# Bucketed attention, routed experts and an ELU block on one core: q and k handed over head dimension first, fp32 projection in four 32-column products

## The chip, the cores and the metric

The kernel runs on one core of one Trainium2 chip. The metric is the device time of one execution in microseconds (us). Lower is better. Profiles come from one execution of their own, which has a time and, inside it, a span from the first to the last profiled instruction.

## What is computed

Three stages follow one another. The change touches the first.

```
# attention: batch 2, 8 heads, 768 tokens, head dimension 64; proj is 64 x 6
q_bits = (einsum('bhsd,dk->bhsk', q, proj) > 0);  k_bits likewise
q_bucket = sum(q_bits * 2**arange(6));            k_bucket likewise
mask   = q_bucket[:, :, :, None] == k_bucket[:, :, None, :]
scores = where(mask, q @ k.T / 8, -1e9)
attn   = exp(scores - max) / (sum + 1e-9)
out    = attn @ v
# then: 1536 tokens routed to one of 8 experts (512 -> 1024 -> 512, relu, two gates)
# then: x @ w_in (2048 wide), ELU, @ w_out
```

A query sees only the keys of its own bucket, so each sign of a projection matters: it is worked out to fp32 precision.

## The kernel before

**Attention, head by head.** There are 16 heads (batch times heads). A head's 768 tokens are six tiles of 128. Six scores tiles `m` are made per head, each 128 queries by 768 keys in two halves of 384 columns, into the PSUM pairs `pair_s` and `pair_t` in turn (`scores`, four products of 384 columns). DVE takes the row maximum (`row_max`), ACT the exponential (`exp_rows`), PE turns the result in six 128x128 transposes into `pair_u` (`turn_exps`), ACT and DVE copy half of it each (`copy_t0`, `copy_t1`), and `times_v` multiplies with v. `times_v` is fp32 and its stationary operand has 64 columns: two heads' halves go to columns 0 to 63 and 64 to 127 of the array, product by product in turn, and each fp32 product shows as two records in the profile. `last` turns the result back and multiplies the routing gates in.

**Masks.** The bucket mask rides in the scores product: rows 64 to 127 of `q_a` and `k_a` hold a one-hot code of the bucket (of `k_a` times 2^60), rows 0 to 63 hold q and k. The second pair, `q_b` and `k_b`, adds what rounding to the fast fp32r format took away: high part times low part.

**Preparation of a head before the change.** q and k arrive token first. PE turns them (`turn_qk`, three transposes each of q and k) into the 384 columns of a bank, with even tiles in partitions 0 to 63 and odd ones in 64 to 127. ACT makes the high part (`split_hi`), DVE the low part (`split_lo`), POOL copies both to where the scores need them (`place_hi`, `place_lo`, ten copies of 64x384). PE projects (`project`: two fp32r products of 128 columns each for q and for k), ACT moves half of it (`keep_low`), DVE compares with zero (`sign`), PE makes the code (`code`), DVE and ACT write the mask rows (`mask_even`, `mask_odd`).

**Order.** Every engine has its queue written out by hand, in groups `n`, three per head (`part` 0, 1, 2). In group `n` stand the scores of `m_s = 2(n-3)` and `m_s+1`, the turning of `m_e = 2(n-4)` and `m_e+1`, the preparation of head `g = n//3` and the `times_v` of the head two back. An instruction waits for semaphores; what stands behind it on its engine waits with it. Heads 0 and 1 are prepared ahead of the loop. In groups 24 to 47, DVE also makes the high part of the first expert's weights (line 1003), and POOL the low part (`w_lo`). SP issues the loads and the stores of the rows.

**After attention** come routing (one chain of small steps), 19 slots of expert products, and the ELU block. The change leaves all this as it was, but for one wait and for the bank in which the last head's rows stand.

Of the kernel before, what the change touches and what calls it, by code (L numbers as in the profile page):

```python
# [22 lines left out]
ALU = mybir.AluOpType  # L23
# [8 lines left out]
P = 128  # L32
# [36 lines left out]
COPIES = 5  # L69
WARM_UP = (7, 6)  # L70
# [13 lines left out]
_WIDTHS = [("ident", P), ("popcount", 1), ("unmatched", 1), ("minus_pop", 1), ("pattern", P), ("tri", P), ("ones", P),  # L84
# [11 lines left out]
def constants():  # L96
# [11 lines left out]
    pattern = np.zeros((P, P))  # L108
    for side in range(2):
        pattern[side * BIT_K:side * BIT_K + NBITS, side * BUCKETS:(side + 1) * BUCKETS] = 2.0 * bits - 1.0  # L110
    put("pattern", pattern)
# [16 lines left out]
def program(nc, q, k, v, proj, w_gate, w_ogate, w1, w2, w_in, w_out, const, out):  # L128
    with ExitStack() as ctx:
# [31 lines left out]
        with ExitStack() as att:  # L161
# [10 lines left out]
            raw = sb("raw", [P, 2, 2, J, D])  # L172
            q_a = sb("q_a", [P, 2, S], F32R)
            k_a = sb("k_a", [P, 2, S], F32R)
            q_b = sb("q_b", [P, 2, S], F32R)
            k_b = sb("k_b", [P, 2, S], F32R)
            x_lo = sb("x_lo", [P, 2, HALF], F32R)
            bits = sb("bits", [P, 2, HALF], BF16)
            nmax = sb("nmax", [P, 2, J])
            proj2 = sb("proj2", [P, NBITS])  # L180
            pat = sb("pat", [P, P])
            pat_bf = sb("pat_bf", [P, P], BF16)
            proj_w = sb("proj_w", [P, 3, P], F32R)
            low_sb = sb("low_sb", [P, 2, HALF])
# [75 lines left out]
        u_bank = lambda u: bank_a if u == HEADS else bank_b  # L260
# [19 lines left out]
        prep_bank = lambda u: bank_b if u in (1, 3) else bank_a  # L280

        def tiles(x, g, odd):
            return x[:, g % 2, :].rearrange("p (j two n) -> p two j n", two=2, n=P)[:, odd]

        def turned(bank):
            return bank[:, 0:HALF].rearrange("p (j n) -> p j n", n=P)
# [3 lines left out]
        s_raw = [[sem(f"s_raw{i}{x}") for x in "qk"] for i in range(2)]  # L290
        s_vld = [sem(f"s_vld{i}") for i in range(4)]
        s_setup = sem("s_setup")
        s_tqk = sem("s_tqk")
        s_hi = sem("s_hi")
        s_lo = sem("s_lo")
        s_cp, s_cpa = sem("s_cp"), sem("s_cpa")
# [4 lines left out]
        s_low = sem("s_low")  # L301
        s_code = sem("s_code")
        s_both = sem("s_both")
        s_pwh, s_pw = sem("s_pwh"), sem("s_pw")
# [89 lines left out]
        copies = lambda u: COPIES * max(u, 1) + 1  # L394
# [4 lines left out]
        def _(sp):  # L399
# [8 lines left out]

            def load_head(g):
                if g >= 5:  # L410
                    store_rows(g - 5)
                if g >= 2:
                    sp.wait_ge(s_tqk, 2 * (g - 2) + 2)
                for n, x in enumerate((q, k)):
                    sp.dma_start(raw[:, g % 2, n], rows(x, g)).then_inc(s_raw[g % 2][n], 16)
                if g >= 4:
                    sp.wait_ge(s_av, g - 2)
                if g >= 2:
                    load_v(g)

            def load_v(g):
                sp.dma_start(v_nat[:, g % 4], rows(v, g)).then_inc(s_vld[g % 4], 16)

            load_head(0)
            sp.dma_start(pat[:, :], const[:, slice(*COL["pattern"])]).then_inc(s_pat, 16)
            load_head(1)
            sp.dma_start(cst[:, P:], const[:, P:]).then_inc(s_cst, 16)
            load_v(0)
            load_v(1)
# [17 lines left out]
            for u in range(HEADS - 5, UNITS):  # L447
                store_rows(u)
# [20 lines left out]
        def _(pool):  # L469
# [24 lines left out]
            def place_hi(g, c):  # L494

                u = 2 * g + c
                if g >= 2:
                    pool.wait_ge(s_sc, J * (g - 1))
                if g >= 3:
                    pool.wait_ge(s_x, g - 2)  # L500
                pool.wait_ge(s_cp, copies(u - 1))
                pool.wait_ge(s_hi, u + 1)
                if c == 0:
                    hi = tiles(q_b, g, 0).bitcast(F32)
                    pool.tensor_copy(tiles(q_b, g, 1)[0:D], hi[D:P]).then_inc(s_cp, 1)
                    pool.wait_ge(s_cp, copies(u - 1) + 1)
                    pool.tensor_copy(tiles(q_a, g, 1)[0:D], hi[D:P]).then_inc(s_cp, 1)
                    pool.wait_ge(s_cp, copies(u - 1) + 2)
                    pool.tensor_copy(tiles(q_a, g, 0)[0:D], hi[0:D]).then_inc(s_cp, 1)
                else:  # L510
                    hi = tiles(k_b, g, 1).bitcast(F32)
                    pool.tensor_copy(tiles(k_b, g, 0)[D:P], hi[0:D]).then_inc(s_cp, 1)
                    pool.wait_ge(s_cp, copies(u - 1) + 1)
                    pool.tensor_copy(tiles(k_a, g, 0)[0:D], hi[0:D]).then_inc(s_cp, 1)
                    pool.wait_ge(s_cp, copies(u - 1) + 2)
                    pool.tensor_copy(tiles(k_a, g, 1)[0:D], hi[D:P]).then_inc(s_cp, 1)

            def place_lo(g, c):

                u = 2 * g + c  # L520
                lo = turned(x_lo[:, c, :]).bitcast(F32)
                pool.wait_ge(s_lo, u + 1)
                pool.wait_ge(s_cp, copies(u) - 2)
                if c == 0:
# [1083 lines left out]
```

## Time and profile before

| | |
|---|---|
| time, median of 3 runs | 789.18 us (788.76 to 789.18) |
| profiled execution: time, and its span | 789.62 us, 787.8 us |
| attention (to the first routing step) | about the first 261 us of the span |
| PE busy over the span | 98% |
| DVE, ACT, POOL busy over the span | 58%, 47%, 43% |

The time is the span and about 1.8 us around it. PE's busy share is high all along the span; whether another engine makes it wait is seen only in the chain of waits and in the small gaps, not in the share.

### The profile page before, as it was taken

How to read it: one execution, taken by the hardware profiler on the slowest of the kernel's cores; microseconds unless marked ns; L12 is line 12 of the kernel's file. 1: busy time of each engine (PE TensorE's matmuls, PEld its weight loads, DVE VectorE, ACT ScalarE, POOL GpSimd, SP SyncE). 2: the span in 40 equal slices, each digit the busy share in tenths (PEclk: the TensorE clock that was granted, in tenths of full speed). 3: DMA queues.
4: the chain of work that ended last, by engine and by line, in shares of the span. 5: the costliest groups of instructions: out<-in, count | busy, mean ns of one | idle time of the engine just before them, and what ended most of it. 6: DMA issues, size and time to landing. Idle time of an engine off the chain costs nothing.

```text
span 787.8 us, 12747 instructions
## 1 busy us (share of the span) xinstructions
PE 772.6 (98%) x4269; PEld 646.3 (82%) x4269; DVE 453.6 (58%) x805; ACT 372.9 (47%) x702; POOL 340.7 (43%) x340
## 2 busy tenths in 40 slices
PE   8999999999999899999999999999999999999997
PEld 6777777787776688888888888899899889989985
DVE  7877878888885655454454544669336316513720
ACT  6787887888776243224432340057227206503610
POOL 4344344656562389798777981134210010000000
PEclk9999999999999999999999999999999999999999
DMA  6022332321110288567465640530010010000000
GB/s 200 22 64 68 110 92 68 88 62 41 42 32 21 50 300 271 182 230 239 154 222 172 229 161 28 174 121 1 28 53 1 14 54 14 0 14 28 1 14 27
DMA packets 41805, 72.68 MB, mean 92 GB/s; under 512 B 18768, under 2 KB 25168, under 8 KB 41744
## 3 DMA queue, kind: packets, MB, share of 16 engines
q10 hardware_dynamic: 9456, 31.53, 12.2%
q1 hardware_dynamic: 28848, 29.06, 11.8%
q0 software_dynamic: 3440, 11.28, 4.3%
q8 instruction: 38, 0.62, 0.3%
q14 instruction: 23, 0.19, 0.1%
HBM read 60.57 MB, written 11.28 MB: 91 GB/s over the span
## 4 chain that ended last, share of the span: by engine, by line
PE 63%; issue 28%; DVE 4%; POOL 2%; ACT 2%; DMA 0%; POOLq 0%; DVEq 0%; ACTq 0%
PE pair_s L1480 13%; PE pair_t L1495 13%; PE bank_b L1305 8%; PE pair_u L1290 7%; PE pair_s L1279 5%; PE pair_t L1279 4%; PE pair_u L1459 2%; PE bank_a L1243 2%; PE bank_b L1325 1%; PE bank_a L1257 1%; POOL out L642 1%; PE pair_s L1532 1%; DVE g_lo L1222 1%; PE bank_a L1265 1%; POOL y_raw L636 1%
## 5 line engine op out<-in xcount | busy, mean ns | idle before, releaser
L472 POOL TENSOR_TENSOR w_part<-w_raw,w_part 128x1024 fp32r<-128x1024 f32 x80 | 190.1, 2414 | 57.4 <-ACT w_part L750 56.7
L750 ACT ACTIVATE w_part<-w_raw 128x1024 fp32r<-128x1024 f32 x72 | 73.8, 1054 | 133.8 <-PE pair_t L1495 101.2
L1582 PE MATMUL pair_t<-w_part,g_hi 128*128 128x512 f32 x384 | 118.9, 391 | 0.3 <-POOL w_part L472 0.3
L1480 PE MATMUL pair_s<-w_part,xs_t 128*128 x456 | 108.7, 394 | 0.3 <-DVE xs_t L1100 0.3
L1495 PE MATMUL pair_t<-w_part,hid_t 128*128 x456 | 109.0, 394 | 0.0
L642 POOL DMA_INDIRECT out<-o_sb,token x12 | 11.8, 986 | 208.5 <-DVE o_sb L1192 208.5
L1480 PEld LDWEIGHTS pair_s<-w_part,xs_t 128*128 128x128 f32 x456 | 84.3, 188 | 17.6 <-issue 0.8
L1495 PEld LDWEIGHTS pair_t<-w_part,hid_t 128*128 128x128 f32 x456 | 84.4, 189 | 16.8
L857 ACT ACTIVATE elu<-elu 128x384 f32<-128x384 f32 x64 | 33.6, 525 | 123.1 <-DVE elu L1212 122.9
L1582 PEld LDWEIGHTS pair_t<-w_part,g_hi 128*128 128x128 f32 x384 | 71.6, 188 | 15.1 <-issue 0.7
L1290 PE MATMUL pair_u<-first,exps 128*128 128x128 f32 x564 | 77.5, 273 | 0.3 <-ACT exps_t L708 0.2
L1582 PE MATMUL pair_t<-w_part,g_lo 128*128 128x512 f32 x192 | 74.9, 390 | 0.0
L1532 PE MATMUL pair_u<-y_t,w_part 128*128 128x384 f32 x384 | 69.3, 334 | 0.3 <-DVE elu L1217 0.3
L1532 PE MATMUL pair_s<-y_t,w_part 128*128 128x384 f32 x384 | 69.3, 335 | 0.0
L1290 PEld LDWEIGHTS pair_u<-first,exps 128*128 128x128 f32 x564 | 65.9, 141 | 3.2 <-ACT exps L699 1.0
L1532 PEld LDWEIGHTS pair_u<-y_t,w_part 128*128 128x128 f32 x384 | 66.8, 188 | 0.7 <-DVE elu L1217 0.6
L1532 PEld LDWEIGHTS pair_s<-y_t,w_part 128*128 128x128 f32 x384 | 66.9, 188 | 0.2
L1305 PE MATMUL bank_b<-exps_t,v_nat 128*64 128x384 f32 x360 | 64.7, 494 | 0.9 <-ACT rows_sb L731 0.9
L1118 DVE CAST hid_t<-pair_u 128x512 fp32r<-128x512 f32 x38 | 26.0, 685 | 67.2 <-PE pair_u L1459 67.2
L903 DVE TENSOR_REDUCE nmax<-pair_s 128x1 f32<-128x768 f32 x48 | 45.8, 954 | 18.0 <-PE pair_s L1279 17.0
L932 DVE COPY exps_t<-pair_u 128x384 f32<-128x384 f32 x94 | 51.5, 548 | 6.4 <-PE pair_u L1290 5.8
L708 ACT ACTIVATE exps_t<-pair_u 128x384 f32<-128x384 f32 x94 | 46.0, 489 | 13.0 <-PE pair_u L1290 11.3
(233 smaller groups left out, 1208.8 us busy)
## 6 DMA issues: line engine op xcount, KB each, us to landing
w_raw<-in_moe_w ACTq DMA_DIRECT2D x48, 512.0 KB, 6.1
w_raw<-in_moe_w SPq DMA_DIRECT2D x16, 512.0 KB, 5.5
ys_sorted<-ys SPq DMA_DIRECT2D x19, 256.5 KB, 3.4
w_raw<-in_moe_w_in ACTq DMA_DIRECT2D x8, 512.0 KB, 6.6
raw<-in_q SPq DMA_DIRECT2D x16, 192.0 KB, 3.8
raw<-in_k SPq DMA_DIRECT2D x16, 192.0 KB, 3.7
v_nat<-in_v SPq DMA_DIRECT2D x16, 192.0 KB, 2.6
x_rows<-rows_sb SPq DMA_DIRECT2D x32, 96.0 KB, 2.4
```

Source lines behind the costliest of these rows:

```text
L472: pool.tensor_tensor(chunk_of(w_part, n, 1, c), w_raw[n % 2][c][:, :], chunk_of(w_part, n, 0, c).bitcast(F32), ALU.subtract).then_inc(s_wl ...
L708: act.activation(turned_tile(m, slice(0, JH)), exps_pair(m)[:, 0, 0:HALF].rearrange("p (j n) -> p j n", j=JH), ACT.Copy).then_inc(s_t0, 1)
L750: act.activation(chunk_of(w_part, n, 0, c), w_raw[n % 2][c][:, :], ACT.Copy).then_inc(s_whi, 1)
L903: dve.tensor_reduce(nmax[:, g % 2, qt:qt + 1], score_pair[m % 2][:, :, 0:HALF], AX.XY, ALU.max, negate=True).then_inc(s_mx, 1)
L932: dve.tensor_copy(turned_tile(m, slice(JH, J)), exps_pair(m)[:, 1, 0:HALF].rearrange("p (j n) -> p j n", j=JH)).then_inc(s_t1, 1)
L1279: mm = pe.matmul(score_pair[m % 2][:, h, 0:HALF], a[:, g % 2, t], b[:, g % 2, h * HALF:(h + 1) * HALF], start=first, stop=not first)
L1290: mm = pe.transpose(exps_pair(m)[:, part, n * P:(n + 1) * P], exps[:, m % 4, kt * P:(kt + 1) * P], ident)
L1305: mm = pe.matmul(u_bank(u)[o * D:(o + 1) * D, 0:HALF], v_nat[:, (u - 1 + o) % 4, j, :], turned_half(2 * u - 1 + o)[:, j], start=j == 0, st ...
L1480: mm = pe.matmul(pair_s[:, h, :], xs_t[:, xp, c * P:(c + 1) * P], w_part[:, bass.ds(par, 1), wp, a:a + 512], start=c == 0 and xp == 0 and ...
L1495: mm = pe.matmul(pair_t[:, s % 2, :], hid_t[:, hp, c * P:(c + 1) * P], w_part[:, bass.ds(par, 1), wp, a:a + DM], start=c == 0 and n == 0, ...
L1532: mm = pe.matmul(hidden_bank[n % 4][:, 0:NB], w_in_p[:, wp, c, f * P:(f + 1) * P], y_t[:, yp, c, :], start=c == 0 and m == 0, stop=c == CD ...
L1582: mm = pe.matmul(pair_t[:, t % 2, :], gp[:, f, j * P:(j + 1) * P], w_out_p[:, wp, f, :], start=f == 0 and m == 0, stop=f == FT - 1 and m == 2)
```

## The change

q and k are handed to the kernel transposed, head dimension in front and tokens in the order that the tiles want (`x.reshape(B, H, P, J, D).transpose(0, 1, 4, 3, 2)`). SP loads each of them twice per head, to partitions 0 to 63 and to 64 to 127. The transposes on PE, and `split_hi`, `split_lo` and `keep_low`, are gone. DVE makes the high parts of q and k in one copy of 128x768 each (`high`); POOL scales k (`raw`, 128x768), copies two high parts and subtracts two low parts (64x768 each). The projection is four plain fp32 products with a 32-column stationary operand and 64 rows, one each for the halves of q and k, into partitions 0, 32, 64 and 96 of one bank; one `sign` follows for q and k together. `q_a`, `k_a`, `q_b` and `k_b` have three buffers in place of two. `scores` of a group stand together in all three parts. The high part of the first expert's weights goes from DVE to ACT in halves. The last head's unit has `bank_a`.

```
-            raw = sb("raw", [P, 2, 2, J, D])
-            q_a = sb("q_a", [P, 2, S], F32R)
-            x_lo = sb("x_lo", [P, 2, HALF], F32R)
+            raw = sb("raw", [P, 2, 2, S])
+            q_a = sb("q_a", [P, 3, S], F32R)
...
-            def turn_qk(g, c):
-                for n in range(JH):
-                    mm = pe.transpose(prep_bank(u)[:, n * P:(n + 1) * P], raw[:, g % 2, c, 2 * n:2 * n + 2, :].rearrange("p j d -> p (j d)"),
-                                      ident)
...
-                parts = ((0, hi), (1, hi), (0, lo)) if g <= 1 else ((2, hi), (0, lo))
-                for n, (w, x) in enumerate(parts):
-                    mm = pe.matmul(prep_bank(u)[:, 0:HALF], proj_w[:, w, :], x, start=n == 0, stop=n == len(parts) - 1)
+            def project(g):
+                    masks = {1: 2, 2: 3}
+                    pe.wait_ge(s_ks, g)
+                    pe.wait_ge(s_raw[g % 2][0], 16 * (g // 2 + 1))
+                    pe.wait_ge(s_mq, masks[g] if g in masks else 2 * g)
+                    pe.wait_ge(s_mk, masks[g] if g in masks else 2 * g)
+                for i in range(4):
+                    mm = pe.matmul(bank_a[i * BIT_K:(i + 1) * BIT_K, 0:HALF], proj_w[:, :],
+                                   raw[0:D, g % 2, i // 2, i % 2 * HALF:(i % 2 + 1) * HALF], start=True, stop=True)
+                mm.then_inc(s_bits, 1)
...
+            def load_qk(g, n, to):
+                sp.dma_start(raw[to, g % 2, n], (q, k)[n][g // H, g % H]).then_inc(
+                    (s_raw if to == top else s_low)[g % 2][n], 16)
...
+            def place_q(g):
+                pool.wait_ge(s_ks, g)
+                pool.wait_ge(s_hia if g == 1 else s_hi, 2 if g == 1 else 2 * (g - 2) + 1)
+                pool.tensor_copy(q_a[top, g % 3, :], q_b[top, g % 3, :].bitcast(F32)).then_inc(s_cp, 1)
+                pool.wait_ge(s_cp, prepared(g - 1) + 1)
+                pool.tensor_tensor(q_b[low, g % 3, :], raw[low, g % 2, 0, :], q_b[low, g % 3, :].bitcast(F32),
+                                   ALU.subtract).then_inc(s_cp, 1)
...
+                pool.tensor_scalar(raw[:, g % 2, 1, :], raw[:, g % 2, 1, :], SCALE, None, ALU.mult).then_inc(s_ks, 1)
+                place_q(g)
+                place_k(g)
...
+            def high(g, c):
+                dve.tensor_copy((q_b, k_b)[c][:, g % 3, :], raw[:, g % 2, c, :]).then_inc(s_hi if g else s_hid, 1)
...
+            def sign(g):
+                dve.wait_ge(s_bits, g + 1)
+                dve.tensor_scalar(bits[:, :], bank_a[:, 0:HALF], 0.0, None, ALU.is_gt).then_inc(s_sgn, 1)
...
-                    if 1 <= u < HEADS:
+                    if 1 <= u < HEADS - 1:
                         pe.wait_ge(s_fr, u)
...
+            pe.wait_ge(s_x, HEADS)
```

**PE's queue, groups of one head.** The head whose `times_v` stands here is in its first and second part; `L1257` is the projection, `L1243` the turning of q or k, `L1265` the code, `L1305` is `times_v`. From the third part of the head before to `times_v`, before the change:

```order
L1325 MATMUL bank_b<-last_w,u_sb 128x160 x3
L1290 MATMUL pair_u<-first,exps 128x128 x6
L1243 MATMUL bank_a<-first,raw 128x128 x3
L1279 MATMUL pair_s<-k_a,q_a 128x384 x2
L1279 MATMUL pair_s<-k_b,q_b 128x384 x2
L1279 MATMUL pair_t<-k_a,q_a 128x384 x2
L1279 MATMUL pair_t<-k_b,q_b 128x384 x2
L1290 MATMUL pair_u<-first,exps 128x128 x6
L1257 MATMUL bank_a<-q_b,proj_w 128x384
L1257 MATMUL bank_a<-x_lo,proj_w 128x384
L1305 MATMUL bank_b<-exps_t,v_nat 64x384 x6
L1265 MATMUL bank_a<-bits,pat_bf 128x384
```

The same place after the change, where `L1155` is the projection of q and k:

```order
L1228 MATMUL bank_b<-last_w,u_sb 128x160 x3
L1191 MATMUL pair_u<-first,exps 128x128 x6
L1155 MATMUL bank_a<-raw,proj_w 32x384 x4
L1180 MATMUL pair_s<-k_a,q_a 128x384 x2
L1180 MATMUL pair_s<-k_b,q_b 128x384 x2
L1180 MATMUL pair_t<-k_a,q_a 128x384 x2
L1180 MATMUL pair_t<-k_b,q_b 128x384 x2
L1191 MATMUL pair_u<-first,exps 128x128 x6
L1206 MATMUL bank_b<-exps_t,v_nat 64x384 x6
L1191 MATMUL pair_u<-first,exps 128x128 x6
L1166 MATMUL bank_a<-bits,pat_bf 128x384
```

The four projection products stand where the turning stood, between two products of the whole array, and the code has moved behind the second turning of the part.

**DVE's queue, second and third part of a head, after the change** (`L860` is `copy_t1`, `L838` is `row_max`, `L831` is `high` of k for the next head, `L852` is `mask_even`, `L866` and `L867` are `inverse`):

```order
L860 COPY exps_t<-pair_u 128x3x128
L838 TENSOR_REDUCE nmax<-pair_s 128x1
L838 TENSOR_REDUCE nmax<-pair_t 128x1
L860 COPY exps_t<-pair_u 128x3x128
L831 CAST k_b<-raw 128x768
L852 TENSOR_SCALAR k_a<-bank_a,first 64x384
L866 TENSOR_SCALAR den<-den 128x6
L867 RECIPROCAL den<-den 128x6
L860 COPY exps_t<-pair_u 128x3x128
L838 TENSOR_REDUCE nmax<-pair_s 128x1
L838 TENSOR_REDUCE nmax<-pair_t 128x1
L860 COPY exps_t<-pair_u 128x3x128 x2
```

Before the change the low part (`L895`), the sign (`L915`) and the mask stood at these places, and a row maximum of the third part was drawn into the second.

**POOL's queue, one head after the change** (`L532` scales k, the next four lines are `place_q` and `place_k`, the last three `rows_of`):

```order
L532 TENSOR_SCALAR raw<-raw 128x768
L505 CAST q_a<-q_b 64x768
L507 TENSOR_TENSOR q_b<-raw,q_b 64x768
L514 CAST k_a<-k_b 64x768
L516 TENSOR_TENSOR k_b<-raw,k_b 64x768
L488 TENSOR_TENSOR rows_sb<-rows_sb,den 128x6x16
L495 TENSOR_TENSOR logit<-logit,rows_sb 128x96
L496 TENSOR_TENSOR rows_sb<-rows_sb,den 128x6x64
```

Before, ten copies of 64x384 stood in the place of the first five, and `rows_of` stood ahead of them.

## Rows read from the trace of the kernel before

**Rows 1.** The page: span; busy time, its share, instructions.

```profile
span 787.8 us, 12747 instructions
PE 772.6 (98%) x4269; PEld 646.3 (82%) x4269; DVE 453.6 (58%) x805; ACT 372.9 (47%) x702; POOL 340.7 (43%) x340
```

**Rows 2.** Chain that ended last, within attention: start us, length us, engine, line.

```profile
21.88 0.98 PE pair_s L1279 x4
...
36.49 0.52 PE bank_a L1243 x3
...
206.80 0.70 PE pair_s L1279 x4
...
208.19 0.66 PE pair_u L1290 x6
208.85 0.35 PE bank_a L1257 x2
209.20 2.09 PE bank_b L1305 x12
211.29 0.27 PE bank_a L1265
...
213.63 0.33 PE bank_a L1243 x3
...
216.70 0.90 PE pair_s L1279 x4
...
219.29 0.28 PE bank_a L1265
...
220.24 0.82 PE bank_b L1325 x6
...
221.72 0.52 PE bank_a L1243 x3
...
241.52 0.81 PE pair_u L1290 x6
```

**Rows 3.** Busy time by engine, one head's period.

```profile
206.28:221.72 15.44, 15.44 (x104) 11.78 (x103) 12.74 (x21) 12.34 (x27) 9.20 (x14) 1.00 0.11 28
```

**Rows 4.** Timeline of one `times_v`: its first weight loads, its products.

```profile
214.54 0.20 PEld L1305 LDWEIGHTS bank_b<-exps_t,v_nat 128*64 128x64 f32 x4 [0.17 <-issue]
214.54 2.16 PE L1305 MATMUL bank_b<-exps_t,v_nat 128*64 128x384 f32 x12
```

**Rows 5.** Timeline: a DVE copy within SBUF and the POOL copies beside it.

```profile
215.83 0.50 POOL L516 CAST k_a<-k_b 64x384 fp32r<-64x384 f32 x1
215.94 0.94 DVE L1003 CAST w_part<-w_raw 128x1024 fp32r<-128x1024 f32 x1
216.46 0.78 POOL L527 CAST k_b<-x_lo 64x384 fp32r<-64x384 f32 x1
```

**Rows 6.** Groups by line: count, busy us, mean ns, idle before.

```profile
L472 POOL TENSOR_TENSOR w_part<-w_raw,w_part 128x1024 fp32r<-128x1024 f32 x80 | 190.1, 2414 | 57.4 <-ACT w_part L750 56.7
L491 POOL TENSOR_TENSOR rows_sb<-rows_sb,den 128x384 f32<-128x384 f32 x14 | 11.6, 831 | 0.0
L708 ACT ACTIVATE exps_t<-pair_u 128x384 f32<-128x384 f32 x94 | 46.0, 489 | 13.0 <-PE pair_u L1290 11.3
```

**Rows 7.** Timeline: two row maxima, one behind the other.

```profile
208.00 0.95 DVE L903 TENSOR_REDUCE nmax<-pair_s 128x1 f32<-128x768 f32 x1
208.86 0.95 DVE L903 TENSOR_REDUCE nmax<-pair_t 128x1 f32<-128x768 f32 x1
```

**Rows 8.** Timeline of the end of attention.

```profile
251.07 0.56 ACT L731 ACTIVATE rows_sb<-bank_b 128x480 f32<-128x480 f32 x1
251.78 2.16 PE L1305 MATMUL bank_b<-exps_t,v_nat 128*64 128x384 f32 x12 [0.87 <-ACT rows_sb L731]
260.91 1.33 ACT L744 ACTIVATE rows_sb<-bank_b,den 128x64 f32<-128x64 f32 x6 [0.95 <-DVE lg_part L1015]
263.26 0.22 PE L1426 MATMUL bank_a<-onehot,tri_bf 128*128 128x104 bf16 x1
```

More of the change, by code:

```diff
@@ L68 @@
 GROUP_S, GROUP_E = 3, 4
-COPIES = 5
-WARM_UP = (7, 6)
+COPIES = 4
+WARM_UP = (7, 10)
 BIT_K = 32
@@ L107, in constants @@
     bits = (np.arange(BUCKETS)[None, :] >> np.arange(NBITS)[:, None]) & 1
[L108 to L111, printed above, removed]
+    pattern = np.zeros((P, 2, P))
+    for x in range(2):
+        for side in range(2):
+            a = (2 * x + side) * BIT_K
+            pattern[a:a + NBITS, x, side * BUCKETS:(side + 1) * BUCKETS] = 2.0 * bits - 1.0
+    put("pattern", pattern.reshape(P, 2 * P))
     put("popcount", np.tile(bits.sum(0), 2)[:, None])
@@ L391, in load_ends @@
                     for e in range(first, last)}
-        copies = lambda u: COPIES * max(u, 1) + 1
+        prepared = lambda g: COPIES * g + 1
         shares = lambda u: 2 * (u + 1)
@@ L553, in _ @@
[L553 to L573 removed]
+            top, low = slice(0, D), slice(D, P)
@@ L584, in _ @@
                         pool.wait_ge(s_twice, 2 + o)
-                if g >= 9:
-                    pool.wait_ge(s_cp, copies(2 * g + 1))
-                    w_lo(0, g - 9)
-            pool.wait_ge(s_cp, copies(2 * HEADS - 1))
-            for c in range(HEADS - 9, NCH):
-                w_lo(0, c)
-            for g in range(HEADS - 3, HEADS - 1):
-                rows_of(g)
+                if g >= 4:
+                    rows_of(g - 4)
+                if g >= 10:
+                    w_lo(0, g - 10)
+            rows_of(HEADS - 4)
+            w_lo(0, HEADS - 10)
+            rows_of(HEADS - 3)
+            w_lo(0, HEADS - 9)
+            rows_of(HEADS - 2)
             pool.wait_ge(s_reach, 1)
@@ L963, in _ @@
             row_max(3)
-            sign(1, 1)
+            high(2, 1)
+            sign(1)
             copy_t1(1)
@@ L1390, in _ @@
                     turn_exps(m_e)
-                if g < HEADS and part == 0:
-                    project(g, 0)
                 if n == 3 * HEADS + 3:
                     turn_exps(m_e + 1)
-                if g == 2 and part == 0:
+                if g < HEADS and part == 1:
+                    code(g, 1)
+                if g == 2 and part == 1:
                     times_v_alone(0, 0, 0)
@@ L1398, in _ @@
                     times_v(g - 2, part)
-                if part == 1 and m_s + 2 < J * HEADS:
-                    scores(m_s + 2)
                 if n == 3 * HEADS + 4:
```

429 lines of the change are left out of this document (150 added, 279 removed).

## The prediction

> **What bounds the kernel now.** I read the page first: PE is busy for 772.6 us of a span of 787.8 us [rows 1]. That alone does not say that PE is never kept waiting, so I took the chain of waits through attention next. From head to head it repeats: the turning of the next q stands at 36.49 us, and twelve heads later at 221.72 us [rows 2], so a head takes (221.72 - 36.49) / 12 = 15.44 us. In one such head DVE has 12.74 us of work, ACT 12.34 and POOL 9.20, at a granted clock of 1.00 [rows 3]. The chain there is PE's rows end to end: PE bounds attention, and what is taken off PE's queue is gained, as long as DVE and ACT deliver in time.
>
> The parts of a head on PE, from [rows 2]: six scores tiles at 0.70, six turnings of exponentials at 0.66, two `times_v` at 2.09, `last` 0.82; for the preparation two turnings of q and k at 0.52 and 0.33, two projections at 0.35, two codes at 0.27 and 0.28. Some of these hold a wait. Four products of 384 columns take 0.70, so one takes 0.17: each code row has 0.10 too much. The turning of 0.52 has 0.19 more than the one of 0.33. And the scores behind a `times_v` take 0.90, not 0.70: leaving the 64-column shape costs 0.20 before scores, 0.10 before a code, and 0.15 before transposes (0.81 against 0.66, the row at 241.52). Sum: 6x0.70 + 6x0.66 + 2x2.09 + 0.82 + 0.85 + 0.70 + 0.55 + 0.20 = 15.46, against 15.44.
>
> **What is removed.** Per head, the turnings with their wait, 0.85, and the projections, 0.70. The code of k stood 0.28 where 0.17 is its work; its sign is now made a part earlier, so 0.11 of wait goes. Together 1.66 us.
>
> **What is added on PE.** Four fp32 products of 384 columns, each in a column group of its own. This shape isn't in the trace; `times_v` is its nearest row. Its six products are twelve records. The stretch of 2.16 us ends with the last record's own length (the group's mean is near 0.49), so the starts spread over 1.67 us: 1.67 / 5 = 0.33, so five steps, six moments; and the weights of four records are loaded at once, within 0.20 us, so that the second group need not wait for the first [rows 4]. Twelve records at six moments is two at each: the two column groups run side by side from the first record on, 0.32 per half product (0.17 x 2 for a product of twice the passes). One product costs 0.64, alone or beside its neighbour; `times_v` is 3 x 0.64 = 1.92 and 0.17 for entering. By this row the bounds for the four products are 0.64 (all side by side) and 4 x 0.64 = 2.56 (none). I take 0.64, since nothing in the row shows the second group paying for the first. With 0.17 for entering and 0.20 for leaving into scores [rows 2], the projection costs 1.01 us a head; the bounds are 1.01 and 2.93. The Trainium skill (TensorEngine Tiling (Array Packing), Key Properties) says that a change of tiling mode drains the engine, which speaks against one more visit per head; the 0.17 and the 0.20 are what this trace shows of it, and they are in the sum.
>
> Leaving `times_v` costs 2 x 0.15 (transposes follow) in place of 0.10 + 0.20: nothing.
>
> **What could newly keep PE waiting.** I laid DVE's and ACT's queues beside PE's for one head: a row maximum starts 0.86 behind the one before it [rows 7], a copy of 384 columns takes 0.49 on ACT [rows 6], and I take 0.55 on DVE. Two places are tight. First, the masks of q wait for the code, which now closes the first part; behind `mask_odd` in ACT's queue stands the copy that the next part's first turning needs. The mask is an ACT instruction of the copy's size: with some 0.15 for each of three hand-overs, 0.17 + 2 x 0.49 + 0.45 = 1.6 us pass from the code's start, against 0.17 + 1.40 of code and scores on PE. I charge 0.06. Second, the third part has little work on PE: from the end of its first scores, DVE does two row maxima and a copy before the second turning's last half can start, against scores 0.70, turning 0.66, `last` 0.82 and half a turning 0.33 = 2.51 on PE. The DVE side is 0.2 to start, 0.86, 0.86 [rows 7] and 0.55 = 2.47. I charge nothing, but any extra work on DVE there goes into PE's time.
>
> DVE's own sum: two low parts and one of two signs (0.55 each, 384 columns) go, two copies of 128x768 come. A 128x1024 copy took 0.94 [rows 5], so each lies between nothing and 0.94; either end leaves DVE's 12.74 us near or under where it was [rows 3]. ACT loses four copies of 384 columns, 0.49 each [rows 6], and gains two of 512 columns in eight heads. POOL: two subtractions of 64x768, between 0.83 and 2.41 each (the 384 and the 1024 column rows) [rows 6], say 1.8; two copies, between 0.50 [rows 5] and 1.0; the scaling, between 0.50 and 2.41, say 1.0; `rows_of` 1.6 (0.83 of it for the 384 columns [rows 6]) and in eight heads `w_lo` 2.4. That is 10.6 us with the middle values and 13.2 with the upper ones, under the 14.9 of a head. It is work for the head after next's scores, so POOL hides behind PE. SP's extra loads have a whole head of room.
>
> The copy at 215.94 and POOL's copy at 216.46 show one more thing: POOL's took 0.78 where its like took 0.50, and it ended 0.36 after DVE's did; DVE's in turn began while POOL's 0.50 was running [rows 5]. One waits for the other. The Trainium skill (SBUF — State Buffer, section on the engine ports) says that DVE and GpSimd share a port pair by exclusive lock; the trace agrees, by the 0.28. In the new order POOL waits for DVE's `high` of q and again of k before it goes on, so they seldom meet. I charge nothing here; it is a rival.
>
> **The sum.** Per head: 15.44 - 1.66 + 1.01 + 0.06 = 14.85, a gain of 0.59. Heads 2 to 14 stand ahead of a projection in the loop: 13 x 0.59 = 7.7 us. In head 15's period no next head is prepared: before, that saved 0.52, now it saves 1.01, so it gains 1.1. At the end, `times_v` of the last unit waited 0.87 us for `copy_rows` to free its bank [rows 8]; it has a bank of its own now, which gives 0.9. The new wait ahead of the routing product costs nothing: ACT's rows end at 262.24, the product starts at 263.26 [rows 8]. It would cost if those rows came over 1 us later.
>
> At the start, the loop's first scores begin at 21.88 us [rows 2]. Now the projection needs only the loads and its weights and no turning, but behind it DVE and POOL pass four instructions of 64x768 or 128x768 to each other before scores can begin, and twice the bytes are loaded. The bounds are 1.5 us sooner (no turning, no splitting) and 2 us later (two POOL subtractions exposed in head 1). I take 0.3 sooner.
>
> Sum: 7.7 + 1.1 + 0.9 + 0.3 = 10.0 us, so the profiled execution goes from 789.62 to 779.6 us. It was 0.44 above the median of 789.18, so the median comes to 779.2; some waits of 0.05 or so that I could not see are likely, and I say 780.0.
>
> **The rivals.**
> - *Column groups wait for one another in program order (slower).* The two halves of a fp32 product stand ahead of the next group's first half. If halves start only in order, the four products take 5 steps of 0.32 = 1.6 us, not 0.64: 13 x 0.96 = 12.5 more, 792.5 us. It decides against the change from 0.64 + 10.0/13 = 1.4 us a projection on. Against it: by the same rule `times_v` would have seven starting moments and spread 6 x 0.32 = 1.92 us, and it spreads 1.67 [rows 4]. For it: only two groups are seen there, not four. The Trainium skill (TensorE: Matmul & The Clock Gate, Part 3) states this rule, that products start and end strictly in program order; the row speaks against it. Chance 0.11. If none run side by side at all, 2.56 each, it is 25 more: 805 us, chance 0.03. Two at a time, 1.28 each: 8.3 more, 788.3 us, chance 0.04.
> - *The DVE copies meet POOL's instructions.* A copy held until a POOL subtraction ends costs up to 1.8; where it falls in the second part, DVE has 0.4 us to spare before its row maximum is due in the third. Some 0.3 to 0.5 a head would come back: 13 x 0.4 = 5, 785 us. For it: the 0.28 of [rows 5]; against: POOL waits for these very copies. Chance 0.13.
> - *The start is worse than thought.* Head 1's low parts are late and the loop starts 2 us later: 782.5 us. Chance 0.09.
> - My forecast, 777 to 783: chance 0.60.
>
> **How the numbers follow.** A measurement of this kernel tells about 0.2%, 1.6 us, from no change. Faster, under 787.6: forecast, port and start, 0.82, less a little for port and start together: 0.81. The two-at-a-time case falls within 0.2%: 0.05. Slower: 0.14. The range from 776 to 788 holds the forecast, the port and the start, and leaves the slower case out (0.14) and a little below.
>
> **What would show it.** In the trace after: a head's period of 14.85 us between two projections; eight records of the projection whose starts fall into two moments 0.32 apart; a projection row of about 0.8 in the chain and 0.9 for the scores behind it; no DVE or ACT entries in the chain of a middle head; the `high` copies near 0.5, and POOL's rows under 11 us a head. It is wrong if the projection's starts are spread over five moments or more, if the chain has row maxima in each third part, or if the loop's first scores come after 23 us.

## The result, and the profile after

The changed kernel takes 792.05 us (median, 791.81 to 792.46); the kernel before, run beside it, 789.18. The ratio is 1.0038, 95% interval 1.0025 to 1.005: slower by a small but measurable amount, where 780.0 and faster had been forecast, with 788 as the upper end of the range. The profiled execution took 792.07 us, with a span of 790.3 us, 2.5 more than before [rows 1].

The page after: span, then busy time, its share and instructions.

```profile
span 790.3 us, 12377 instructions
PE 766.2 (97%) x4237; PEld 628.2 (79%) x4237; DVE 440.8 (56%) x776; ACT 352.7 (45%) x658; POOL 374.3 (47%) x258
```

PE has 6.4 us less work than before, as was meant, and the span is longer. So PE waits now where it did not. Where, is seen by cutting attention at places that both chains have.

**The projection is what was forecast.** Windows on PE's records that write `bank_a`, around one projection: stretch, length, busy time and number of records that lie in it, granted clock, DMA share, GB/s.

```profile
178.37:178.42 0.05, 0.04 (x4) 1.00 0.00 0
178.42:178.72 0.30, 0.30 (x4) 1.00 0.00 0
178.72:178.77 0.05, 0.05 (x8) 1.00 0.00 0
```

Four records begin within 0.05 us, none in the next 0.30, and the other four within 0.05 behind that. These are the two moments of the prediction: all four column groups run side by side. In the chain of the changed kernel the head's period is then read from one projection to the next:

```profile
56.71 0.78 PE bank_a L1155 x8
57.49 0.91 PE pair_s L1180 x4
...
64.93 0.16 PE bank_a L1166
...
71.61 0.78 PE bank_a L1155 x8
```

The projection takes 0.78, the scores behind it 0.91, the code 0.16, and the period is 71.61 - 56.71 = 14.90 us against a forecast of 14.85 and 15.44 before [rows 3]. Nothing but PE stands in the chain between them. But only four periods are like this.

**Heads 8 to 14 are not.** Windows of one head's period, early and late, with the columns of [rows 3] (PE, its weight loads, DVE, ACT, POOL, granted clock, DMA share, GB/s):

```profile
56.71:71.61 14.90, 14.90 (x104) 10.70 (x108) 11.55 (x19) 10.34 (x23) 8.70 (x9) 1.00 0.38 109
199.91:215.44 15.53, 15.00 (x103) 10.61 (x102) 11.56 (x19) 11.39 (x24) 11.25 (x9) 1.00 0.07 18
```

The late one is 15.53 us long, 0.09 more than before, and PE is busy for 15.00 of it: 0.53 is waiting. ACT has 1.05 more work, POOL 2.55 more. Neither is near the period. The chain shows which piece of work it is:

```profile
199.91 0.17 PE bank_a L1166
...
200.13 0.58 issue
200.71 0.63 ACT w_part L696
...
201.36 0.50 ACT exps_t L652
...
201.99 0.85 PE pair_u L1191 x6
```

PE makes the code (L1166). ACT waits for it, writes the mask (L630; the chain books its 0.58 us as issue), then converts half a chunk of the first expert's weights (L696, 0.63), then copies the turned exponentials (L652), for which PE's next turning (L1191) waits. The 0.63 stands in the middle of the one place that the prediction had called tight on ACT, and it is there in the eight heads in which weights are converted.

**Head 3.** The chain at the end of the first part of head 3, in a period of 15.91 us (one projection at 40.80, the next at 56.71):

```profile
47.56 1.12 DVE tri_bf L913
...
48.95 0.48 DVE exps_t L860
...
49.48 0.55 PE pair_u L1191 x3
```

Three constants for routing are converted on DVE in this head alone, ahead of the copy that PE's turning waits for. They stood there before too, and head 3 then took as long as any other (its scores and those of head 4 at 37.01 and 52.45 us, 15.44). What has changed is the length of the first of them. Timeline after, then before:

```profile
46.76 1.84 POOL L507 TENSOR_TENSOR q_b<-raw,q_b 64x768 fp32r<-64x768 f32 x1
...
47.56 1.12 DVE L913 CAST tri_bf<-cst 128x128 bf16<-128x128 f32 x1
```

```profile
42.52 0.52 DVE L996 CAST tri_bf<-cst 128x128 bf16<-128x128 f32 x1
```

It begins while POOL's subtraction runs and ends 0.08 us behind it (48.68 against 48.60), as the one before ended 0.08 behind a POOL copy of 0.50 (from 42.46). The other two constants take 0.21 each. So of the 1.0 us that head 3 takes more than the next (15.91 - 14.90), 0.60 is DVE held longer by POOL. The other 0.4 would be the place alone; that split is an estimate.

**The start.** The chain from the loads to the first projection inside the loop's even beat:

```profile
2.61 5.27 DMA pat<-in_const
...
7.93 1.06 POOL pat_bf L520
...
11.78 2.16 POOL raw L532
...
17.88 1.83 POOL k_b L516
...
20.15 2.14 POOL raw L532
...
22.32 0.04 DVE k_b L831
...
22.79 0.55 DVE bits L845
...
27.89 0.80 PE pair_s L1180 x4
...
40.80 0.78 PE bank_a L1155 x8
41.58 0.55 PE pair_s L1180 x2
```

From 7.93 to 22.32 the chain is POOL's rows nearly all the way, with one ACT copy of 0.85 and short hand-overs between them. The scaling of k, put at 1.0 us in the prediction, takes 2.1; DVE's high part of k (L831) waits for the second scaling, and the sign, a copy and a row maximum wait behind it on DVE. The loop's first scores begin at 27.89, not at 21.88 [rows 2]. The forecast had called 23 the point from which it is wrong.

**The end.** `times_v` of the last unit, which had waited 0.87 us [rows 8], follows the turning at once:

```profile
253.55 0.76 PE pair_u L1191 x6
254.31 2.09 PE bank_a L1206 x12
```

**The sum of the differences**, from the two chains at the same instructions (after minus before):

| stretch | forecast | measured |
|---|---|---|
| to the loop's first scores (27.89 against 21.88) | -0.3 | +6.0 |
| head 2, from there to the scores at 41.58 against 37.01 | -0.6 | -1.4 |
| head 3 (15.91 against 15.44) | -0.6 | +0.5 |
| heads 4 to 7 (4 x (14.90 - 15.44)) | -2.4 | -2.2 |
| heads 8 to 14 (7 x (15.53 - 15.44)) | -4.1 | +0.6 |
| head 15 | -1.1 | -0.2 |
| the last units | -0.9 | -0.8 |
| sum | -10.0 | +2.5 |

+2.5 is the difference of the spans. The misses add up to 12.5 us: 5.5 up to head 3, 1.1 in head 3, 0.2 in heads 4 to 7, 4.7 in heads 8 to 14, 0.9 in head 15, 0.1 at the end. Head 15 has a weights conversion too (0.63 at 231.76 in the chain); the other 0.3 there was not traced.

### The profile page after: what moved, and what is told of

Same layout as the page of the kernel before. It is cut to its first block, busy times and chain, and to the rows that moved or that the text cites. A ratio compares the mean times of both kernels' runs of the same rounds, so it can differ in the third digit from the quotient of the medians.

```text
span 790.3 us, 12377 instructions
## 1 busy us (share of the span) xinstructions
PE 766.2 (97%) x4237; PEld 628.2 (79%) x4237; DVE 440.8 (56%) x776; ACT 352.7 (45%) x658; POOL 374.3 (47%) x258
## 4 chain that ended last, share of the span: by engine, by line
PE 59%; issue 28%; DVE 4%; POOL 4%; ACT 2%; DMA 1%; POOLq 0%; SPq 0%; DVEq 0%
PE pair_s L1369 13%; PE pair_t L1384 13%; PE pair_u L1191 8%; PE bank_b L1206 7%; PE pair_s L1180 4%; PE pair_t L1180 3%; PE pair_u L1348 2%; PE bank_b L1228 1%; PE bank_a L1155 1%; POOL out L605 1%; PE pair_s L1421 1%; DVE g_lo L1132 1%; POOL y_raw L599 1%; DMA pat<-in_const 1%; ACT w_part L696 1%
## 5 line engine op out<-in xcount | busy, mean ns | idle before, releaser
L1191 PEld LDWEIGHTS pair_u<-first,exps 128*128 128x128 f32 x564 | 62.7, 140 | 32.4 <-ACT exps L643 18.6
L1191 PE MATMUL pair_u<-first,exps 128*128 128x128 f32 x564 | 81.0, 278 | 6.0 <-ACT exps_t L652 4.6
L652 ACT ACTIVATE exps_t<-pair_u 128x384 f32<-128x384 f32 x94 | 46.0, 489 | 49.9 <-PE pair_u L1191 49.6
L860 DVE COPY exps_t<-pair_u 128x384 f32<-128x384 f32 x94 | 51.8, 552 | 23.8 <-PE pair_u L1191 23.4
L1206 PE MATMUL bank_b<-exps_t,v_nat 128*64 128x384 f32 x336 | 60.4, 494 | 0.0
L838 DVE TENSOR_REDUCE nmax<-pair_s 128x1 f32<-128x768 f32 x48 | 45.8, 954 | 18.9 <-PE pair_s L1180 17.5
```

The costliest lines, as they stand in the source:

```text
L652: act.activation(turned_tile(m, slice(0, JH)), exps_pair(m)[:, 0, 0:HALF].rearrange("p (j n) -> p j n", j=JH), ACT.Copy).then_inc(s_t0, 1)
L838: dve.tensor_reduce(nmax[:, g % 2, qt:qt + 1], score_pair[m % 2][:, :, 0:HALF], AX.XY, ALU.max, negate=True).then_inc(s_mx, 1)
L860: dve.tensor_copy(turned_tile(m, slice(JH, J)), exps_pair(m)[:, 1, 0:HALF].rearrange("p (j n) -> p j n", j=JH)).then_inc(s_t1, 1)
L1191: mm = pe.transpose(exps_pair(m)[:, part, n * P:(n + 1) * P], exps[:, m % 4, kt * P:(kt + 1) * P], ident)
L1206: mm = pe.matmul(u_bank(u)[o * D:(o + 1) * D, 0:HALF], v_nat[:, (u - 1 + o) % 4, j, :], turned_half(2 * u - 1 + o)[:, j], start=j == 0, st ...
```

## The experiments

Three causes were read from the trace. Each of the first three kernels takes one away and nothing else; the fourth takes all three. The kernel before took 788.93 us beside them (788.88 beside experiments 5 to 8, 788.98 beside 9 to 11).

**1. The weights ahead of the mask on ACT** (theory: the place of the 0.63 us costs it; rival: ACT's larger sum of work).

```
+                if 8 <= g < 8 + NCH and part == 0:
+                    first_hi(g - 8, part)
                 if g < HEADS and part < 2:
                     mask_odd(g, part)
                 if g >= 2 and part == 1:
                     copy_u(g - 2)
-                if 8 <= g < 8 + NCH and part < 2:
+                if 8 <= g < 8 + NCH and part == 1:
                     first_hi(g - 8, part)
```

> Changed kernel with one line moved: in heads 8 to 15, ACT makes the first half of a weight chunk's high part ahead of the mask of q (where it sits idle 1.07 us in the first part of a head), not behind it. Theory: that half chunk, 0.63 us, stands in front of the copy that PE's next turning waits for, once a head; so a head's period falls from 15.53 to 14.90 us and the time from 792.05 by 8 x 0.63 = 5.0 to 787.0 us. Rival: ACT simply has too much to do in these heads (11.39 us of 15.53), the place doesn't matter: period 15.4 to 15.5, time 791.5 to 792.

Measured: 787.58 us, ratio to before 0.9982 (0.9973 to 0.9991). 4.5 us came back by moving one ACT instruction in eight heads. Windows of one period of this kernel, with the same columns:

```profile
191.07:206.06 14.99, 14.99 (x105) 10.63 (x108) 11.55 (x19) 11.38 (x25) 11.26 (x10) 1.00 0.33 80
```

ACT and POOL are as busy as in the late row above (11.38 and 11.26), and PE waits for nothing. The place was the cost, not the amount. Head 15, from its first scores to the first behind it, takes 14.21 us (221.84 to 236.05), where the changed kernel took 14.74 (225.83 to 240.57).

**2. DVE's high part of k later in the start** (theory: it drags what stands behind it on DVE through POOL's 2.13 us).

```
             row_max(3)
-            high(2, 1)
             sign(1)
...
             copy_t1(2)
+            high(2, 1)
```

> Changed kernel with one line moved: ahead of the loop DVE makes the high part of head 2's k behind everything else, not ahead of head 1's sign. Theory: that copy waits for POOL's scaling until 22.3 us and holds sign, copy and row maximum behind it (DVE idle 2.30 us, PE 2.10 us); head 1's sign moves from 22.8 to about 20.0 us, the loop's first scores from 27.7 to about 25.0, the time falls by 2.6 to 789.4 us. Rival: POOL's chain (its low parts of head 1 end at 19.7) or the loads set the loop's start, the wait only moves: under 0.8 us gained.

Measured: 789.77 us, ratio 1.0005 (0.9995 to 1.0014), 2.3 us less than the changed kernel. In its chain the first regular projection comes 2.24 us sooner than at 40.80:

```profile
38.56 0.78 PE bank_a L1155 x8
```

**3. The routing constants ahead of the mask on DVE**, where the mask's wait for the code covers them.

```
+                if n == 9:
+                    dve.wait_ge(s_cst, 16)
+                    dve.tensor_copy(tri_bf[:, :], cc("tri"))
+                    dve.tensor_copy(ones_bf[:, :], cc("ones"))
+                    dve.tensor_copy(iota_bf[:, :], cc("iota"))
                 if g < HEADS and part < 2:
                     mask_even(g, part)
-                if n == 9:
...
```

> Changed kernel with three DVE copies of routing constants in head 3 moved ahead of the mask of q, where DVE is idle 1.2 us. Theory: behind the mask they held the copy that PE waits for (0.80 us idle at 49.5): head 3's period falls from 15.91 to 14.9 us, the time by 1.0 to 791.0 us. Rival: the first of them meets POOL's copy wherever it stands (1.12 us where its like before took 0.52), and holds the mask now: period 15.5 to 15.9, time 791.6 to 792.

Measured: 791.44 us, ratio 1.004 (1.0026 to 1.0054). By the times alone that is hardly told from the changed kernel. The trace tells it: head 3's projections stand at 40.75 and 55.66, a period of 14.91 us and not 15.91, so the 1.0 us is gone. The three conversions together still take 1.11 us (45.62 to 46.73), as the last of them now takes 0.84 beside a POOL copy; the mask behind them starts at 46.89, when the code is there, so they hold nothing. From its chain:

```profile
55.66 0.44 PE bank_a L1155
```

**4. All three.**

> Changed kernel with the three moves of the other runs together. Theory: they are in different stretches and add up, 5.0 + 2.6 + 1.0 = 8.6 us: 783.4 us, faster than the kernel before by 0.7%. Rival: one of them only makes room for the next wait; then 785 to 788 us.

Measured: 784.34 us, ratio 0.9945 (0.9932 to 0.9957): 7.7 us less than the changed kernel, where the three alone gave 4.5, 2.3 and 0.6. They add up to 7.4, within the scatter of the runs, so they are separate causes. This kernel is faster than before by 4.6 us. Its scores of the first regular head begin at 39.21: the start is still 2.2 us behind before. The next four went after that.

**5. ACT's table load out of the way**, in the kernel of experiment 4.

```
+            act.wait_ge(s_zero, 3)
+            act.activation(u_sb[0:D, 0:1], last_w[0:D, 0, 1, 0:1], ACT.Copy)
             act.wait_ge(s_raw[0][1], 16)
```

> The kernel of e4_three (784.34 us, first scores at 11.79 us of its trace) with one more ACT instruction of one element ahead of its wait for k, so that the 1.28 us of table load pass while nothing else can be done. Theory (the table load holds the copy k_b, 8.07, but pat_bf on POOL, 7.70 to 8.10, is due at the same time): the first code stays near 8.2, first scores near 11.7, 784.3 us. Rival (the table load alone is what is late): k_b near 6.8, code near 7.0, first scores near 10.5, 783.1 us.

Measured: 784.14 us, ratio 0.9932 (0.9918 to 0.9945); code at 8.43, first scores at 11.97. The load of 1.28 us now passes at 2.87, and k's high part is there 1.3 us sooner, but nothing later moves: the patterns were due at the same time. As the theory had it.

**6. The patterns sooner, and on DVE.** As 5, and:

```
             sp.dma_start(proj_w[:, 0:NBITS], proj).then_inc(s_proj, 16)
-            load_qk(0, 0, low)
             sp.dma_start(pat[:, :, :], const[:, slice(*COL["pattern"])]...
+            load_qk(0, 0, low)
...
-            pool.tensor_copy(pat_bf[:, :, :], pat[:, :, :]).then_inc(s_setup, 1)
...
             sign(0)
+            dve.wait_ge(s_pat, 16)
+            dve.tensor_copy(pat_bf[:, :, :], pat[:, :, :]).then_inc(s_setup, 1)
```

> As s1_table, and the sign patterns are loaded one transfer earlier and cast on DVE, not on POOL. Theory: the table load and the patterns together are what holds the first code; it comes near 7.1, the mask q_a on POOL near 8.8 to 10.4, first scores near 10.7, and the loop starts 1.1 us sooner: 783.2 us. Rival (from the first scores to the loop it is POOL's own scaling of 2.13 us and its subtractions of 1.8 us, which begin with the loads of the low parts and not with the first scores): first scores near 10.7 but the loop's first as in e4_three, 784.3 us.

Measured: 784.06 us, ratio 0.9938 (0.9924 to 0.9951). Neither line of the expectation came out. The code came at 8.18, not 7.1: the cast now stands behind the sign on DVE. Timeline of this kernel:

```profile
7.33 0.71 DVE L872 CAST pat_bf<-pat 128x256 bf16<-128x256 f32 x1
...
8.18 0.48 PE L1169 MATMUL bank_a<-bits,pat_bf 128*128 128x384 bf16 x1 [1.40 <-DVE pat_bf L872]
...
10.91 2.15 POOL L529 TENSOR_SCALAR raw<-raw 128x768 f32<-128x768 f32 x1 [0.73 <-DMA raw<-in_k]
...
11.68 0.62 PE L1183 MATMUL pair_s<-k_a,q_a 128*128 128x384 f32 x2
```

And yet the first regular head's scores began at 38.49, 0.72 sooner than in experiment 4, where the first scores had moved by only 0.11 (11.79 to 11.68). What had moved by 0.72 is POOL's first scaling (11.63 to 10.91). So the loop's start follows POOL's row of work and not the first scores, as far as this one step of 0.72 us shows. The gain does not show in the median. The profiled execution is the slowest of its five (785.62 us); from 250 to 300 us it has a granted clock of 0.97, where experiment 4 has 1.00.

**7 and 8. Two warm-up products in place of ten** ahead of the first scores, in the kernel of experiment 4 and in that of 6 (`WARM_UP = (7, 2)`; the output does not depend on them). The changed kernel has ten of these products there, the kernel before six; this too is part of the change.

> The kernel of e4_three with 2 of the 10 warm-up products ahead of the first scores, not 10 (the output is not touched by them). Theory: they end 0.1 us before the mask of q that the first scores wait for anyway, so nothing is gained by leaving them out, and PE's products after them are spaced wider for longer (0.32 us for one of 384 columns instead of 0.17): 784.3 to 785.3 us. Rival (the warm-up holds the first scores): 783.3 us or less.

Measured: 786.86 us, ratio 0.9968 (0.9956 to 0.9979), 2.5 us above experiment 4: the direction of the theory, and more than its range. Two of the eleven executions (783.41 and 784.29 us) lost nothing. In the profiled one (786.93) the loss is in the start: the first regular projection comes at 41.03 us against 38.43 in experiment 4.

> s2_pat and s3_warm together. Theory: 2.9 us of warm-up would end near 10.6, about when the mask of q is ready, so leaving 8 of them out adds nothing to s2_pat: 783.2 us. Rival (they hold the scores once the patterns come sooner): 0.5 us or more below s2_pat, 782.6 us.

Measured: 785.43 us (783.92 to 787.08), ratio 0.9963 (0.9949 to 0.9976), 1.4 above experiment 6: neither 783.2 nor 782.6. The profiled execution is the fastest of the five and lost nothing (first regular projection at 37.78, 37.72 in experiment 6). Timeline of the second scores, experiment 4 first, then 7:

```profile
15.82 0.58 PE L1182 MATMUL pair_s<-k_a,q_a 128*128 128x384 f32 x2 [2.36 <-ACT exps L643]
...
16.59 0.82 PE L1193 MATMUL pair_u<-first,exps 128*128 128x128 f32 x6
```

```profile
15.80 0.98 PE L1182 MATMUL pair_s<-k_a,q_a 128*128 128x384 f32 x2 [1.12 <-ACT exps L643]
...
17.21 1.49 PE L1193 MATMUL pair_u<-first,exps 128*128 128x128 f32 x6
```

From the start of these four scores products to the start of the turning behind them 0.77 us pass in experiment 4 (16.59 - 15.82) and 1.41 in experiment 7 (17.21 - 15.80), with nothing between them in either. In experiment 7 this lasts until about 20 us; in the profiled execution of experiment 8 it is over with the second scores (0.79 us from 15.53 to 16.32). So the loss differs from execution to execution, and by the medians the warm-up is worth its place, though the first scores start no later with it (11.79 us against 11.77).

**9. The projection's products made twice**, in the changed kernel; the output is the same.

```
-                for i in range(4):
+                for i in (0, 1, 2, 3, 0, 1, 2, 3):
```

> The changed kernel with the four products of every projection made a second time (groups 0, 1, 2, 3 and again 0, 1, 2, 3, the same values into the same places). Theory (column groups run side by side, each group is busy 0.64 us for one fp32 product of 384 columns): the projection's 0.78 us become 1.42, of which little is hidden in heads 4 to 14 (16 projections in all, 15 of them on the path): 10 us more than the changed kernel, 802 us, and all eight projections of the trace's first eight records again start within 0.4 us. Rival (products start in program order with their halves, and the 0.78 was an overlap with something else): 1.28 us or more per projection, 811 us or more.

Measured: 801.32 us, ratio 1.0161 (1.0145 to 1.0176). In its chain:

```profile
73.04 1.42 PE bank_a L1155 x16
```

1.42 for sixteen records against 0.78 for eight. One more set of four fp32 products costs 0.64 us.

**10. Four more products, all in column group 0.**

```
-                for i in range(4):
+                for i in (0, 0, 0, 0, 0, 1, 2, 3):
```

> The changed kernel with four more products of every projection, all four into column group 0 and ahead of the four that are kept (same values into the same place). Theory (only products of different column groups run side by side; in one group they follow each other at 0.64 us): 4 x 0.64 = 2.56 us more per projection, 15 on the path and partly hidden nowhere: 38 us more, 830 us. Rival (it isn't the column group that lets them overlap, but the small shape of 64x32 as such): 0.64 us more, as in p_twice: 802 us.

Measured: 830.55 us, ratio 1.0525 (1.0509 to 1.0541). In its chain:

```profile
64.50 3.34 PE bank_a L1155 x16
```

The same number of products as in 9, of the same shape: 2.56 us more, four times 0.64, where another group each had cost 0.64 for the four. The small shape as such does not let them run side by side; different column groups do. A group is also its rows of the bank, so that the four extra products write one place again and again; products of one group into different columns of the bank weren't tried. The same execution shows how far the groups go their own ways. Windows on PE's records that write `bank_a`, in the projection that begins at 81.89:

```profile
83.80:83.84 0.04, 0.04 (x1) 1.00 0.00 0
83.84:83.88 0.04, 0.04 (x5) 1.00 0.00 0
...
84.98:85.28 0.30, 0.30 (x1) 1.00 0.24 55
```

Up to 83.84 one record follows another: the first three products, all of group 0. Then four begin at once. As two of one group never do, they are one of each group: group 0's fourth product and the single ones of groups 1, 2 and 3. Group 0's fifth product, which stands in the program ahead of those three, comes 0.64 later and runs alone at the end. So a product starts ahead of one of another group that stands before it. The signal to the reader does not come ahead with it. It is tied to the last product, of group 3; in the first projection of this execution DVE's sign starts only when all sixteen records have ended (5.21 + 6.61 = 11.82). Timeline:

```profile
5.21 6.61 PE L1155 MATMUL bank_a<-raw,proj_w 64*32 64x384 f32 x16 [1.68 <-DMA proj_w<-in_proj]
...
11.90 0.56 DVE L845 TENSOR_SCALAR bits<-bank_a 128x384 bf16<-128x384 f32 x1 [9.04 <-PE bank_a L1155]
```

**11. The last unit's bank alone**, in the kernel before.

```
-        u_bank = lambda u: bank_a if u == HEADS else bank_b
+        u_bank = lambda u: bank_a if u == HEADS - 1 else bank_b
...
+            pe.wait_ge(s_x, HEADS)
             pe.matmul(ring[0][:, 0:(TILES + 1) * E], tri_bf[:, :], ...
```

> The kernel of before with one part of the change alone: times_v of the last unit writes the bank that the projections no longer need (bank_a), and the routing product waits for the end of the last rows. Theory: the 0.87 us that it waited for copy_rows fall away, and nothing else changes: 788.1 us, 0.9 below before. Rival (the wait only moves to the next thing that needs the last unit's rows, such as the routing product): 789.0 us, no change.

Measured: 788.28 us against 788.98, ratio 0.9992 (0.9983 to 1.0001): the median is down by 0.7, and the interval just holds no change. The trace shows the wait gone; `times_v` follows the turning at once, and the routing product starts 261.74 - 250.17 = 11.57 us behind the first of these rows, where 0.87 of waiting and, in the chain before, 263.42 - 251.78 = 11.64 had stood [rows 8].

```profile
250.17 2.09 PE bank_a L1305 x12
...
261.74 0.06 PE bank_a L1429
```

## Why the prediction was wrong

**What bounds the kernel, and what was removed and added on PE: right.** PE's own work gave 14.90 us a head against 14.85. Projection 0.78 (forecast 0.81), entering and leaving as priced, code 0.16 without its wait. The disputed step, 0.64 for four products side by side, stands: experiments 9 and 10 measure 0.64 for a product of each group and for each further product in one group. The rivals of program order (792.5) and of two at a time (788.3) are out, although the measured time lies almost on the first one's number: a total proves no mechanism. The Trainium skill (TensorE: Matmul & The Clock Gate, Part 3) has products start and end strictly in program order. As a rule on whole products the rows around 178.4 don't speak against it: four start at once and four end together. As a rule on the halves, which the rival made of it, they do. Two records of one group never start at once (in experiment 10 each product of group 0 adds its full 0.64), so the four are one of each group: the first half of the fourth product starts ahead of the second half of the first. And in experiment 10 the starts of whole products don't agree with it either: group 0's fifth starts 0.64 us behind the three that follow it in the program.

**"ACT loses four copies ... and gains two of 512 columns in eight heads": the step that failed in heads 8 to 15.** It was made with sums of busy time, and by them ACT was far from the bound, then as now. The place in the queue was not costed. The prediction had worked out that from code to the copy behind the mask ACT had no slack (0.06 was charged), and it put nothing further there, though the new instruction stands exactly there. 0.63 us in each of eight heads, 5 us; experiment 1 returned 4.5. This was the largest error in the loop.

**"I take 0.3 sooner", with bounds of 1.5 sooner and 2 later: the step that failed in the start, and the largest miss.** It was 6.0 later at the loop's first scores, outside its own bounds, and the rival "the start is worse" was priced too low at 2 us. One part is shown by a run: DVE's `high` of k waits in front of other work (2.3 us, experiment 2). Two more are read from the chain, with no run that takes them away: the scaling on POOL takes 2.13, not 1.0 (the bound of 0.50 to 2.41 held it, but the middle was taken), and POOL's work for head 2 is on the path there, as no head hides it. Only the sum over a whole head's POOL work was checked against the period, which is right in the loop and says nothing of the start. In the group of POOL's instructions by line after the change:

```profile
L532 POOL TENSOR_SCALAR raw<-raw 128x768 f32<-128x768 f32 x15 | 32.0, 2130 | 0.4
L507 POOL TENSOR_TENSOR q_b<-raw,q_b 64x768 fp32r<-64x768 f32 x15 | 27.5, 1832 | 1.3
L505 POOL CAST q_a<-q_b 64x768 fp32r<-64x768 f32 x15 | 12.7, 843 | 34.5 <-DVE q_b L831 34.4
```

The subtraction, 1.83, and the copy, 0.84, were well placed (1.8, up to 1.0). The sum of 10.6 us for POOL has the copies at their upper value; with 0.75 each it is 10.1. POOL's work in a late head came to 11.25, over the 11 that the forecast allowed, and cost the loop nothing: experiment 1 has 11.26 in a head in which PE never waits.

**"Any extra work on DVE there goes into PE's time": the right worry, in one place of two.** The prediction said it of the third part, and there the loop's chain is PE alone (from 53.08 to the projection at 56.71, say). It did not ask it of the first part, where DVE's copy behind the mask of q is as tight as ACT's. The constants in head 3 stand just there: 1.0 us.

**The rival of DVE's copies meeting POOL's instructions: wrong for `high` in the loop, right elsewhere.** In the loop POOL waits for `high` (34.4 us of idle time of L505 in the row above), as was argued, and `high` takes 0.55 in the middle. But the first routing constant does meet POOL in head 3 (1.12 for 0.52), and in the start `high` does (below). The prediction charged nothing for either.

**The last units: right.** 0.9 forecast, 0.8 measured; experiment 11 shows that it is the bank.

**What stays open.** With the three causes away, the kernel takes 784.3 us and not 780. Of this, the start is 2.2 us behind before (1.5 with experiment 6), where 0.9 ahead had been forecast, and a late head takes 14.97 to 14.99 us in place of 14.85. In the chain of experiment 4 from 24.0 us to the projection at 38.43 nearly all is DVE, and three of its instructions run long beside POOL's: `high` 1.40 (23.93) and 0.88 (28.38) where alone it takes 0.55, and the first `inverse` 1.05 (33.93) where none takes over 0.32 in the changed kernel. That is 1.9 us over, an estimate of what the meetings cost there; no run takes them away.

## What to carry to other kernels

Where a period is filled to a few tenths by one engine, a sum of busy time clears no other engine: lay each new or moved instruction into its queue and ask which waiting instruction it stands behind and who waits for the one after it. An instruction that waits for nothing belongs ahead of one that waits (experiments 1 and 3 are that and nothing more; with experiment 2, which puts a copy that waits for POOL behind work that doesn't, they turned a loss of 0.4% into a gain of 0.5%). The fill of a pipeline is costed by itself, with no cover from a neighbouring head, and an engine that is idle for 6 of a head's 15 us in the loop, as POOL is here, can be the bound there.

## What the hardware showed that was not expected

**Four column groups of fp32 products.** A product of 64 rows, 32 columns and 384 moving columns costs 0.64 us alone, and four cost 0.64 together if each has a column group of its own. The second halves of all four start together, 0.35 us behind the first. A product can start ahead of one of another group that stands before it in the program, while the signal of the last product still comes when all have ended (experiment 10).

**POOL's price goes with the operation and the columns.** For 768 columns, a product with a scalar takes 2.13 us (128 partitions), a copy with cast 0.84 (64) and a subtraction of two operands 1.83 (64). The subtraction of 128x1024 takes 2.41 [rows 6], the same per column with twice the partitions.

**A DVE copy within SBUF that starts during a POOL subtraction ends 0.4 us behind it.** Timeline of experiment 4:

```profile
14.75 1.82 POOL L507 TENSOR_TENSOR q_b<-raw,q_b 64x768 fp32r<-64x768 f32 x1
15.07 1.91 DVE L833 CAST q_b<-raw 128x768 fp32r<-128x768 f32 x1 [0.48 <-DMA raw<-in_q]
```

POOL ends at 16.57, DVE at 16.98, 0.41 later. In experiment 6 the copy at 23.22 takes 1.41 and ends 0.43 behind POOL's subtraction (22.38, 1.82); in experiment 5 the one at 15.34 takes 1.54 and ends 0.41 behind (14.66, 1.81). Alone it takes 0.55. A conversion of 128x128 ends 0.08 behind POOL's subtraction in head 3 (above). The Trainium skill (SBUF — State Buffer, Who interferes with whom) tells of an exclusive lock that whoever comes second waits out in full; these rows agree, in that DVE ends behind POOL each time, by 0.41 to 0.43 for 128x768.

**The granted clock does not tell PE's pace in the start.** The row of experiment 7 from 11.7 to 16.0 us shows a granted clock of 1.00, that is 2.4 GHz, as that of experiment 4 does; yet products of 384 columns are spaced 0.32 us from start to start in experiment 7 and 0.17 in experiment 4. What PE did before differs: ten products without a gap from 8.84 on in experiment 4, two in experiment 7, and then 2.0 us of idle time. The window of experiment 7:

```profile
11.70:16.00 4.30, 3.10 (x9) 2.65 (x10) 2.25 (x3) 2.13 (x4) 4.15 (x3) 1.00 1.02 271
```
